# Spatial mixing in seven products of block sums for batches 1 to 3, and low parts stored in the place of their raw values

## The reference

```python
h = np.maximum(x @ w_in, 0.0)                       # 768 x 1024
u, v = h[..., :512], h[..., 512:]
v_n = (v - mean(v)) / np.sqrt(var(v) + 1e-06)       # over the 512 channels of a token
v_s = np.einsum('ts,bsd->btd', w_spatial, v_n) + b_spatial[None, :, None]
return (u * v_s) @ w_out                            # 768 x 384
```

## Time and profile before

| | us |
|---|---|
| median of 3 runs | 598.52 (597.65 to 598.63) |
| profiled execution | 597.77 |
| its span, first to last instruction | 596.0 |
| PE busy | 582.2 |
| DVE, ACT, POOL busy | 369.4, 237.1, 199.4 |

### The profile page before, as it was taken

One profiled execution on the slowest core, in us unless ns is written; L12 is line 12 of the kernel. 1 busy time (PEld: TensorE's weight loads), 2 busy tenths in 40 slices (PEclk: granted clock), 3 DMA queues, 4 the chain that ended last, 5 costly groups with the idle time before them and its releaser, 6 DMA issues.

```text
span 596.0 us, 11233 instructions
## 1 busy us (share of the span) xinstructions
PE 582.2 (98%) x4631; PEld 554.5 (93%) x4631; DVE 369.4 (62%) x561; ACT 237.1 (40%) x451; POOL 199.4 (33%) x175
## 2 busy tenths in 40 slices
PE   6899899999999999999999999999999999999998
PEld 5788899999999999999999989999999999989997
DVE  7988996877877877778733466747044714371232
ACT  3767555444544534544443228223222313231110
POOL 2565444232432422422321144536023702361130
PEclk9999999999999999999999999999999999999999
DMA  8943212222321420413032280201020010002002
GB/s 303 339 155 123 79 67 68 92 84 67 107 67 68 142 99 29 145 67 108 1 136 89 86 313 0 80 0 54 27 80 1 27 53 1 1 0 81 1 0 81
DMA packets 20403, 49.54 MB, mean 83 GB/s; under 512 B 1664, under 2 KB 15232, under 8 KB 19840
## 3 DMA queue, kind: packets, MB, share of 16 engines
q1 hardware_dynamic: 20352, 48.81, 23.5%
HBM read 39.37 MB, written 9.44 MB: 82 GB/s over the span
## 4 chain that ended last, share of the span: by engine, by line
PE 89%; DVE 5%; ACT 2%; issue 2%; POOL 1%; DMA 0%; DVEq 0%; ACTq 0%
PE psY L471 21%; PE psC L503 6%; PE psY L610 6%; PE psC L430 5%; PE psS L610 4%; PE psF L610 4%; PE psY L587 4%; PE psS L379 3%; PE psY L597 3%; PE psF L413 3%; PE psF L577 3%; PE psY L577 2%; PE psS L587 2%; PE psC L610 2%; PE psS L597 2%; PE psF L597 2%
## 5 line engine op out<-in xcount | busy, mean ns | idle before, releaser
L1133 POOL TENSOR_TENSOR z_lo<-cos_sin,z_hi 128x768 fp32r<-128x768 f32 x23 | 43.7, 1900 | 104.8 <-ACT z_hi L717 104.8
L1199 POOL TENSOR_TENSOR gated_lo<-u_gated,gated_hi 128x384 fp32r<-128x384 f32 x32 | 32.4, 1012 | 123.7 <-ACT gated_hi L837 123.6
L837 ACT ACTIVATE gated_hi<-u_gated 128x384 fp32r<-128x384 f32 x32 | 16.8, 525 | 79.3 <-DVE u_gated L1068 79.3
L1120 POOL TENSOR_TENSOR akq<-akq 128x512 f32<-128x512 f32 x23 | 27.4, 1192 | 58.3 <-DVE akq L896 58.3
L471 PE MATMUL psY<-tok_r_hi,z_hi 128*128 128x384 f32 x126 | 45.5, 361 | 1.1 <-POOL z_lo L1133 1.1
L471 PE MATMUL psY<-tok_r_hi,z_lo 128*128 128x384 f32 x126 | 42.2, 335 | 0.0
L471 PE MATMUL psY<-tok_i_hi,z_lo 128*128 128x384 f32 x126 | 42.2, 335 | 0.0
L471 PE MATMUL psY<-tok_i_hi,z_hi 128*128 128x384 f32 x126 | 42.2, 335 | 0.0
L471 PE MATMUL psY<-tok_i_lo,z_hi 128*128 128x384 f32 x126 | 42.2, 335 | 0.0
L471 PE MATMUL psY<-tok_r_lo,z_hi 128*128 128x384 f32 x126 | 42.1, 334 | 0.0
L885 DVE TENSOR_TENSOR akq<-akq,after 128x512 f32<-128x512 f32 x24 | 41.5, 1731 | 0.9
(11 more groups left out here) (239 smaller groups left out, 1768.3 us busy)
## 6 DMA issues: line engine op xcount, KB each, us to landing
akq<-akq SPq DMA_DIRECT2D x22, 770.0 KB, 4.4
v<-v_in SPq DMA_DIRECT2D x24, 192.0 KB, 4.5
x_dram<-u_f SPq DMA_DIRECT2D x8, 576.0 KB, 3.7
x_raw<-x_dram SPq DMA_DIRECT2D x4, 1152.0 KB, 5.3
out<-ot SPq DMA_DIRECT2D x24, 192.0 KB, 1.9
raw_tok_r<-w_tok_rT SPq DMA_DIRECT2D x6, 384.0 KB, 7.2
raw_tok_i<-w_tok_iT SPq DMA_DIRECT2D x6, 384.0 KB, 8.7
raw_sp<-w_spT SPq DMA_DIRECT2D x1, 2304.0 KB, 9.2
```

The source lines that it names most:

```text
L1133: pool.tensor_tensor(Z[c][1][:], trigs[g % 2][:], f(Z[c][0][:]), ALU.subtract).then_inc(z_lo, 1)
L1199: pool.tensor_tensor(GA[1][:, j, half(h)], ug[h][:, j], f(GA[0][:, j, half(h)]), ALU.subtract).then_inc(g_lo, 1)
```

## The change

Both matrices of the spatial mixing are cut in 2 x 2 blocks: the normalised values into A (token halves and channel halves, 384 x 256), the weights into B (384 x 384). The result's four blocks were eight block products. In batches 1 to 3 they become seven products (`PRODUCTS`), by the scheme of Strassen in Winograd's form: sums S1 to S4 of the values' blocks, made by DVE for each of these batches (`sum_values`, 12 adds of 256 columns; S4 replaces a block in `vt`), and T1 to T4 of the weights' blocks, made once (`sum_weights`, 4 adds of 1152 columns). Four banks for each of two column tiles take the products; three of the seven grow on a bank that holds an earlier product (`GROWS`), after DVE has taken a snapshot of it with the bias added (`take`, `snap`, `SNAP_FREES`). `gate` adds a snapshot in the place of the bias. Batch 0 takes the eight products, block by block in `FIRST_PRODUCTS`, from the same storage.

With it move:

- Low parts lie where the raw values were (`pair`), for the weights, the values and their sums, w_out, x2 and the gated values. So `load_x2` waits for the batch's gate inputs, and on SP it stands behind `store_out` of the batch before; x2 of batch 0 has a place of its own (`x2first`); the bias waits for `x2_low(0)` and w_out for the last channel mixing.
- `vt` has six slots; `relu_v` waits for the mixing of the batch before and no longer for `vn_low`. In batches 1 to 3 nine parts are split in place of six (`VN_ORDER`), after the sums.
- The weights come in four DMAs. ACT makes eight high blocks of 1152 columns (before, six of 768), DVE eight low ones: four before the first gate, four between the gates of batch 0. In batch 0 `sum_weights` stands on DVE ahead of the moments of chunk 2.
- `x2_low` of the next batch moves on DVE from ahead of the gates to a place among them.

```diff
+A11, A12, S2, A22, S3, S1, S4, A21 = range(8)
+B11, B21, T2, T4, T3, T1, B22, B12 = range(8)
+BW, BY, BX, BZ = range(4)
+BANK_OF = (BX, BW, BX, BY, BX, BZ, BZ)
+GROWS = (False, False, True, False, True, False, True)
+SNAP_FREES = {S2: 0, S3: 2, S4: 6}
+PRODUCTS = 7
+BLOCKS = 8
+SNAPS = 8
+FINISHED = ((0, 0), (0, 1), (1, 1), (1, 0))
+FIRST_PRODUCTS = (((A11, B11), (A12, B21)), ((A21, B11), (A22, B21)), ((A21, B12), (A22, B22)), ((A11, B12), (A12, B22)))
+SP_ORDER = (B11, B21, B12, B22, T2, T4, T3, T1)
...
+VN_ORDER = (0, 1, 3, 2, 4, 5, PAIR, PAIR + 1, PAIR + 2)
...
+        def pair(name, shape, hi_at, lo_at):
+            hi, raw, lo = Region(hi_at), Region(lo_at), Region(lo_at)
+            return raw("raw_" + name, shape), [hi(name + "_hi", shape, F32R), lo(name + "_lo", shape, F32R)]
...
+        raw_sp, WS = pair("sp", [BLOCKS, CT, HALF], 0, sp_bytes)
...
+        raw_vn, VN = pair("vn", [CHUNKS, G], small_at, work_at)
...
+        x2raw, X2 = pair("x2", [CT, SEQ], z_at, z_at + x2_bytes)
+        raw_sums, VS = pair("vsum", [CT, 3, G // 2], z_at + 2 * x2_bytes, z_at + 3 * x2_bytes)
...
+        x2first = Region(x_at)("x2_first", [CT, SEQ])
...
+        snap = r("snaps", [2, 2, HALF])
...
+        ug, GA = pair("gated", [GT, SEQ], keep_at + g_bytes, keep_at)
...
             sp.wait_ge(y_made, BATCH * TILES)
-            sp.dma_start(raw_sp[:], w_spT.rearrange("(c p) n -> p c n", p=P)).then_inc(sp_in, 16)
+            w = w_spT.rearrange("(k c p) n -> p k c n", k=2, p=P)
+            sp.dma_start(raw_sp[:, B22], w[:, 1, :, half(1)]).then_inc(sp_in[0], 16)
+            sp.dma_start(raw_sp[:, B12], w[:, 0, :, half(1)]).then_inc(sp_in[0], 16)
+            sp.dma_start(raw_sp[:, B11], w[:, 0, :, half(0)]).then_inc(sp_in[1], 16)
+            sp.dma_start(raw_sp[:, B21], w[:, 1, :, half(0)]).then_inc(sp_in[1], 16)
+            sp.wait_ge(x2_lo, CT)
+            sp.dma_start(bias[:], b_sp.partition_broadcast(P)).then_inc(bias_in, 16)
+            sp.wait_ge(ch_made, BATCH * TILES)
             sp.dma_start(raw_out[:], w_out.rearrange("(c p) n -> p c n", p=P)).then_inc(out_in, 16)
-            sp.wait_ge(u_made, BATCH * TILES)
-            sp.dma_start(bias[:], b_sp.partition_broadcast(P)).then_inc(bias_in, 16)
             store_x2(BATCH - 1, 1)
             def load_x2(b):
-                sp.wait_ge(x2_lo, b * CT)
+                sp.wait_ge(gi_made, b * GN)
                 for h in range(HALVES):
                     sp.wait_ge(stored[h], 16 * (b + 1))
                 sp.dma_start(x2raw[:], x2_dram[b]).then_inc(x2_in, 16)
...
             load_x2(1)
             for b in range(1, BATCH):
+                store_out(b - 1)
                 if b + 1 < BATCH:
                     load_x2(b + 1)
-                store_out(b - 1)
...
-                pe.wait_ge(g_lo, b * GN + GT * (i // (CHUNKS // HALVES) + 1))
+                pe.wait_ge(g_lo, b * GN + (GT if i < CHUNKS // HALVES else GN))
...
+            def factor(k, l, c, i):
+                if k in (S1, S2, S3):
+                    return VS[l][:, c, (S1, S2, S3).index(k), tile(i)]
+                row, at = {A11: (c, i), A12: (CT + c, i), A22: (CT + c, 2 + i), A21: (c, 2 + i), S4: (c, 2 + i)}[k]
+                return VN[l][:, row, tile(at)]
...
+                            pe.wait_ge(vn_lo, p * CT + c + 1)
+                        for m, (l, part) in enumerate(PASSES):
+                            mm = pe.matmul(banks[n % RING][:, 0:HALF], factor(k, l, c, i), WS[part][:, w, c],
+                                           start=(p == 0 and c == 0 and m == 0), stop=(p == 1 and c == CT - 1 and m == 2))
+                mm.then_inc(sp_made, 1)
+            def spatial_product(b, k, i):
+                n = USES.index(("S", b, 2 * BANK_OF[k] + i))
+                if GROWS[k]:
+                    pe.wait_ge(snapped, (b - 1) * SNAPS + SNAP_FREES[k] + i + 1)
+                else:
+                    free2(n)
+                for c in range(CT):
+                    if i == 0 and k in (A11, A12, S2):
+                        part = {A11: 0, S2: PAIR, A12: CT}[k] + c
+                        pe.wait_ge(vn_lo, vn_before(b, part) + 1)
+                    if b == 1 and i == 0 and c == 0:
+                        pe.wait_ge(sp_lo, SP_ORDER.index(k) + 1)
+                    for m, (l, part) in enumerate(PASSES):
+                        mm = pe.matmul(banks[n % RING][:, 0:HALF], factor(k, l, c, i), WS[part][:, k, c],
+                                       start=(not GROWS[k] and c == 0 and m == 0),
+                                       stop=(c == CT - 1 and m == 2), skip_group_check=True)
...
+                if b == 0:
+                    for bank in range(4):
+                        for i in range(2):
+                            first_spatial(bank, i)
+                else:
+                    for k in range(PRODUCTS):
+                        for i in range(2):
+                            spatial_product(b, k, i)
                 if b == 0:
                     pe.wait_ge(out_lo, 1)
...
-            def vn_high(b, i):
-                n = b * CHUNKS + i
-                act.wait_ge(vn_made, n + 1)
-                need(act, sp_made, b * GN)
-                act.activation(VN[0][:, i, :], vt[n % VSLOTS][:], ACT.Copy).then_inc(vn_hi, 1)
+                need(act, sp_made, products_before(b))
+                act.activation(vt[:, i], banks[USES.index(("V", b, i)) % RING], ACT.Relu).then_inc(v_relu, 1)
+            def vn_high(b, part):
+                c = part % CT
+                if b:
+                    act.wait_ge(v_sums, ((b - 1) * CT + c + 1) * 4)
+                    act.wait_ge(sp_made, products_before(b))
+                else:
+                    act.wait_ge(vn_made, part + 1)
+                hi, raw = (VN[0][:, part], vt[:, part]) if part < PAIR else (VS[0][:, c], raw_sums[:, c])
+                act.activation(hi, raw, ACT.Copy).then_inc(vn_hi, 1)
+            def sp_high(k):
+                if k in (T1, T2, T3, T4):
+                    act.wait_ge(t_made, (T3, T1, T2, T4).index(k) + 1)
+                else:
+                    act.wait_ge(sp_in[k in (B11, B21)], 32)
+                act.activation(WS[0][:, k], raw_sp[:, k], ACT.Copy).then_inc(sp_hi, 1)
...
-                need(act, g_lo, n + 1 - GN)
-                act.activation(ug[h][:, j], banks[USES.index(("U", b, i)) % RING][:, 0:HALF],
+                need(act, o_made, b * CHUNKS)
+                act.activation(ug[:, j, half(h)], banks[USES.index(("U", b, i)) % RING][:, 0:HALF],
...
+            def sum_values(b, c):
+                n = ((b - 1) * CT + c) * 4
+                first, second = slice(0, G // 2), slice(G // 2, G)
+                s1, s2, s3 = (raw_sums[:, c, i] for i in range(3))
+                dve.wait_ge(sp_made, products_before(b))
+                dve.wait_ge(vn_made, b * CHUNKS + CT + c + 1)
+                dve.tensor_tensor(s1, vt[:, c, second], vt[:, CT + c, second], ALU.add).then_inc(v_sums, 1)
+                dve.tensor_tensor(s3, vt[:, c, first], vt[:, c, second], ALU.subtract).then_inc(v_sums, 1)
+                dve.wait_ge(v_sums, n + 1)
+                dve.tensor_tensor(s2, s1, vt[:, c, first], ALU.subtract).then_inc(v_sums, 1)
+                dve.wait_ge(v_sums, n + 3)
+                dve.tensor_tensor(vt[:, c, second], vt[:, CT + c, first], s2, ALU.subtract).then_inc(v_sums, 1)
+            def sum_weights(k):
+                if k == T3:
+                    dve.wait_ge(sp_in[0], 32)
+                    dve.tensor_tensor(raw_sp[:, T3], raw_sp[:, B22], raw_sp[:, B12], ALU.subtract).then_inc(t_made, 1)
+                elif k == T1:
+                    dve.wait_ge(sp_in[1], 32)
+                    dve.tensor_tensor(raw_sp[:, T1], raw_sp[:, B12], raw_sp[:, B11], ALU.subtract).then_inc(t_made, 1)
+                elif k == T2:
+                    dve.wait_ge(t_made, 2)
+                    dve.tensor_tensor(raw_sp[:, T2], raw_sp[:, B22], raw_sp[:, T1], ALU.subtract).then_inc(t_made, 1)
+                else:
+                    dve.wait_ge(t_made, 3)
+                    dve.tensor_tensor(raw_sp[:, T4], raw_sp[:, B21], raw_sp[:, T2], ALU.subtract).then_inc(t_made, 1)
+            def sp_low(k):
+                dve.wait_ge(sp_hi, SP_ORDER.index(k) + 1)
+                dve.tensor_tensor(WS[1][:, k], raw_sp[:, k], f(WS[0][:, k]), ALU.subtract).then_inc(sp_lo, 1)
...
+            def take(b, n, k, i, h, place):
+                dve.wait_ge(sp_made, products_before(b) + 2 * k + i + 1)
+                dve.tensor_tensor(snap[:, place, i], product_bank(b, BANK_OF[k], i), bias[:, half(h)],
+                                  ALU.add).then_inc(snapped, 1)
+            def gate(b, n, k=None, taken=None, place=None):
+                h, half_of_columns = FINISHED[n // 2]
+                i = n % 2
+                j = 2 * half_of_columns + i
+                mixed_bank = product_bank(b, n // 2, i)
+                if b == 0:
```

(132 more changed lines are left out.)

102 lines of the change are left out of this document (41 added, 61 removed).

## The result

The kernel with seven products takes **590.63 us** (median of 4 runs, 590.20 to 590.95) where the kernel before, run beside it, takes 598.13 (597.65 to 598.63): a ratio of 0.987, 95% interval 0.9858 to 0.9883. The forecast was 589.2, with a range of 588.2 to 591.8. The direction, the mechanism and the range held. The sum is 1.4 us too low, and most of what follows is about where that went. The profiled execution took 590.33, its span is 588.6 (before 596.0).

The account below looks back on a forecast made before the run. TensorE, busy without waits, was taken as the bound, so time goes by the number of matmuls. The earlier median 598.52 minus 9.36, with every other term hidden or 0, gave 589.2 us, range 588.2 to 591.8.

Parts of the forecast that it names:

- Matmuls removed: Spatial mixing, batches 1 to 3: 126 matmuls each in place of 144, 54 fewer at 0.1733 us, 9.36 us saved.
- Nothing else on TensorE changes in count or shape.: All of TensorE's work outside the removed mixing matmuls: count and shape stay, so no further term in the sum.
- Snapshots and gates: DVE during mixing, batches 1 to 3: no TensorE wait; tightest is S4, with 0.9 us to spare.
- rival B: Batches 1 and 2: x2_low among the snapshots makes them late, 0.5 to 2 us; 590 to 593 us, chance 0.07.
- rival C: Late x2 load holds DVE and eats the whole gain, needing 4.7 us of stall in each of two batches; chance 0.03.
- Sums of the values: Batches 1 to 3 before mixing: 12 DVE adds, 4.5 us, and POOL's low parts stay hidden, 6 us to spare.
- the tail: After batch 3's mixing: gated low parts are ready before the outputs want them, with 1.3 and 2.7 us to spare.
- Batch 0: First mixing: weight sums delay DVE's chain, low weights still ready with one microsecond to spare; taken as 0, bounds to 3 us.
- Overlap of DVE and POOL: Batch 0: DVE loses 0.76 us per us of overlap with POOL, 1.0 us for POOL's first two vn_low.
- rival A: Batch 0: weight sums before the moments stall TensorE at first mixing, 0.7 to 3 us; 590 to 592 us, chance 0.17.
- that part of rival A: Batch 0: whole overlap lost and one more pass meets POOL's work; some 590.5 us, chance 0.05.
- Price of a stall: TensorE throughout the touched stages: a late operand costs all of its lateness.

Follow-up runs that it names:

- experiment 1: The changed kernel with the split w_in 64 bytes lower, where the kernel before has it; 589.75 us, ratio 0.9852; timed again beside the changed kernel, 588.80 us.
- experiment 6: The changed kernel with eight block products in every batch, without value sums and snapshots in batches 1 to 3; 599.52 us, ratio 1.0025 to the kernel before.
- experiment 8: The changed kernel with each of batch 0's four weight sums made twice, delaying DVE; 596.41 us, ratio 0.9977 to the kernel before.
- experiment 7: The changed kernel with the next batch's x2_low ahead of all snapshots on DVE; 599.68 us, ratio 1.0025 to the kernel before.
- experiment 10: The changed kernel with w_in at its old place, seven products in batch 0 too and ACT's gate-input copies first; 595.52 us, ratio 0.9955 to the kernel before.

## Why the prediction was right, and its one wrong term

- **Matmuls removed, 9.36.** Right to the hundredth: 249.84 - 240.48 in experiment 1, and nothing at all with eight products (experiment 6).
- **"Nothing else on TensorE changes in count or shape."** True as it is worded, and the step that failed: from it I priced all other matmuls at their old spacing. The new layout put w_in 64 bytes up, and the 486 matmuls of x with w_in in the late part (72 of `gate_inputs` in each of four batches, 54 of `values` in three and 36 in batch 0) cost 1.22 us more in all. The shift stands in the code: w_in's parts begin at `late_at`, where before they simply followed `raw_in`, 64 bytes lower (the diff ahead leaves that line out). With that term the sum is 590.4, measured 590.63 and 590.17; without it (experiment 1) 589.2 was forecast and 589.75 and 588.80 measured.
- **Snapshots and gates.** Right in detail. Counted from 432.47, x2_low ran from 9.9 to 12.6 (forecast 9.9 to 12.6), S3's first snapshot began at 14.1, S1's first was done at 17.8 and wanted at 18.56 (slack 0.8, forecast 0.9), the last gate ended at 23.9 (23.7). x_hi was complete at 7.3, not 9.1, as the load landed in 4.9 us. Rivals B and C did not come.
- **Sums of the values.** Hidden, as forecast, with a little less room: in batch 1 POOL's last low part is over 32.7 us after the values began (forecast 31), and the mixing starts at 37.6. The chain has no wait in the tail either.
- **Batch 0.** Last norm over at 365.8 (forecast 365.4), B11 at 368.21 (367.7), B21 at 370.59 (369.5), the mixing at 369.76 (368.79; the start of the late part was 0.73 later). The slack of 0.73 to 1.55 is the forecast's "one microsecond", and experiment 8 confirms B11's 1.55. That B21's came out so near (0.73, forecast 0.85) is partly luck: 0.9 us lost beside POOL was not in the sum, and it was made up by a chain that ran a little ahead of the forecast (counted from the start of the late part, ACT's high part of B21 was ready 0.5 earlier) and by w_in's slower products, which put the mixing 0.24 later.
- **Overlap of DVE and POOL.** I took 0.76 us lost per us of overlap, from the earlier trace rows, and left a complete exclusion to rival A. The reading was wrong: I divided DVE's loss of 2.67 by all of POOL's 3.50, but POOL had begun at 371.64 and DVE only at 372.33, so they overlapped for 2.81 us, and the loss is 0.95 of that. The rows after show whole exclusion, in turns. POOL's pass of 352.31 began inside DVE's sum of 352.12, which took its usual 1.36, and ended 1.14 behind it. DVE's next sum began inside that pass and ended 1.22 behind it. The two passes of POOL from 365.60 and the low parts of B11 and B21 follow each other in the same way: 367.00, 368.21, 369.37 and 370.59 are their ends. "SBUF — State Buffer", "Who interferes with whom", of the Trainium skill says that the later one blocks fully; these rows agree, and the one in progress was spared (1.36, and 1.40 against 1.29). DVE lost 1.0 on the sums (forecast 1.0), 1.1 on B11 (1.0) and 0.9 on B21 (none). So both conditions of that part of rival A were met, the whole overlap lost and one more pass that met POOL, but not its price: 1.0 more than in the sum and not 1.7, and TensorE did not wait.
- **Price of a stall.** I counted a late operand at "all of its lateness". Where the wait is some 3 us and over, it costs about half as much again (experiments 7 and 8). That would have moved rival A's and B's times up by some 1.7 a stall at the far end, and C's condition from 4.7 us to 3; no chance depended on it by much.

## What to carry to other kernels

On a TensorE that never waits, removed matmuls are worth their spacing exactly, provided that the work on the others still lands before it is asked for: read each slack from the timeline, and keep the extra sums out of the one stage where there is none. When a change moves buffers, compare the spacing of matmuls that it did not touch, per nine or eighteen in the chain, and keep the distance between two operands' starts at a multiple of 256 bytes until measured otherwise. Where a pass of DVE with two inputs in SBUF begins inside such a pass of POOL, or the other way round, let the later one start at the end of the first. Count a stall of 3 us on TensorE as nearly 5.

## What the runs showed of the hardware that was not expected

- The spacing of back-to-back float32r matmuls depends on how far apart in SBUF its two operands start. With 384 columns it is 0.1733 us at a multiple of 256 bytes, 0.1767 at a remainder of 64 and 0.176 at 128. Nine matmuls with 512 columns take 2.04, 2.06 and 2.10. The remainder of 64 was seen in several profiles; 128, the step of 256 and the shift of everything together rest on one profile each. Why it is so is open, and other remainders, other shapes and the operands of the first two stages weren't tried.
- After waits of 2.9 to 3.9 us TensorE ran at the lower of its two clock levels, 1.2 GHz, with eight to ten matmuls at a spacing of 0.32 us, 1.65 to 1.84 us more in all. So it did after the 2.1 us wait of experiment 10, which came behind four others; after those, of 0.6 to 1.3, it did not.
- A pass of DVE with two inputs in SBUF that begins inside such a pass of POOL waits for its end, however short it is. The pass over a single column, `moments`, takes 0.16 us alone; here it starts 0.11 behind a pass of POOL and ends with it:

```profile
358.07 1.29 POOL L1368 TENSOR_TENSOR vn_lo<-raw_vn,vn_hi 128x512 fp32r<-128x512 f32 x1 [0.34 <-ACT vn_hi L905]
...
358.18 1.20 DVE L1141 TENSOR_TENSOR moments<-moments 128x1 f32<-128x1 f32 x1
```
